# Token-stationary down products of an expert: high parts of four blocks first, their low parts behind

## Chip, cores, metric

One core of a Trainium2 chip runs one program. The metric is device microseconds of one execution; the kernel before takes 435.81 us, the median of 3 runs (434.45 to 435.82).

## What is computed

A linear attention with a per-channel decay feeds a dense two-layer network with a leaky activation, and that feeds a top-1 mixture of 8 experts. The change lies in the last part:

```python
expert_idx = np.argmax(x @ w_gate, axis=1)            # 1536 tokens, 8 experts
...                                                   # up to capacity = 384 tokens an expert
h = np.maximum(np.einsum('ecd,edf->ecf', disp, w1), 0.0)   # d = 384, f = 1024
y = np.einsum('ecf,efd->ecd', h, w2)
out[i] = gate_w[i] * y[expert_idx[i], pos[i]]
```

With these inputs the experts are chosen by 478, 132, 159, 141, 398, 57, 118 and 53 tokens. The first 256 rows of expert 0 are done ahead (the "early" rows), so the expert loop has 128 rows for expert 0, then 132, 159, 141, 384, 57, 118 and 53.

## The kernel before, in words

Every operand of a product is split into a high part (rounded) and a low part (the rest), and a product is three: high by high, high by low, low by high. `wh` and `wl` hold both parts of the weights (W1 in the first 384 columns of a slot, W2 in the other 384; 16 slots, so two experts' worth), `egh` and `egl` those of the hidden activations g.

An expert runs in tiles of 128 tokens, and the number of its rows decides, by branches on every engine, which code runs:

- **One tile** (experts 0, 5, 6, 7): "flipped". `flip_up` (L1604 to L1619) keeps the tokens stationary and gives h by token, 512 columns at once, in two halves; VectorE takes the relu (`flip_relu`, L1190); `flip_turn` (L1622 to L1635) transposes four blocks a half; ScalarE copies them as `egh` (`flip_high`, L843) and VectorE writes `egl` (`flip_low`, L1196, which for tile 0 raises `s_mgl` by four).
- **Two tiles** (experts 1, 2, 3): `expert_ups` (L1555) gives h by channel for 256 tokens in eight steps f, ScalarE takes the relu (`relu`, L790), VectorE the low part (`relu_low`, L1138). Then `expert_down` for tile 1 and for tile 0.
- **Three tiles** (expert 4): the same for tiles 0 and 1, and the third tile flipped.

`expert_down` (L1576 to L1597) is the down product of one tile: for each of the eight blocks f three matmuls of 384 columns, all of one accumulation in one PSUM bank. A block waits for its low part (`s_mgl`, or `s_fl` for the third tile) and for W2's low part (`s_wl2`).

TensorE's program for an expert has two branches one after the other: L1653 (one tile, or else) and L1674 (no third tile, or else). In the first arm of the second branch TensorE also raises a mark for the third tile that is not there:

```python
expert_down(e, 0, range(HF + 1))
pe.wait_ge(s_mgl, e * NFE + NFE + C_MGL)
pe.sem_inc(s_ft[1], 2)
expert_down(e, 0, range(HF + 1, NFE))
```

`s_ft[1]` is "third tile transposed". ScalarE and VectorE run the third tile's copies for every expert of two or three tiles (`flip_high(e, 2)`, L843, waits for that mark; `flip_low(e, 2, half)` behind it), whether there is such a tile or not. Behind `flip_high(e, 2)` ScalarE's queue has, in order: eight copies of W1 of expert e+2 (`split_high1`, L798) with the three scaled copies of y among them (L828), and then the relus of expert e+1 (L790). GpSimd forms W1's low parts from those eight copies (L633) and raises `s_gone` (L643) behind them; VectorE takes the token numbers and gates of the next expert (`keep_meta`, L1159 and L1160), which wait for `s_gone`, and only then the next expert's `relu_low`, W2's low parts (L1145) and the rows of the expert after (`xe_low`, L1151). TensorE's next `expert_down(e, 1)` waits, through `turned`, for two of these `xe_low`, since tile 1's bank holds transposed rows till then.

Of the kernel before, what the change touches and what calls it, by code (L numbers as in the profile page):

```python
# [3 lines left out]
P = 128  # L4


def attention_moe_kernel(nc, att_rk, att_v, decay, bonus, chunks, alpha, w_gate, out, disp,
# [26 lines left out]
    NF = FF // P  # L34
    NFE = FE // P
    SLOTS = 2 * NFE
    assert NF == SLOTS and CAP == GT * P and CT == 6 and PAIRS == KC + 1 and D == KC * PAD and CT == 2 * GT
    W1 = KC * P
    CW = W1 + DM
# [10 lines left out]
    ET = 2  # L50
# [32 lines left out]
    wh = base.take("w_high", [P, SLOTS, CW], f32r)  # L83
    wl_from = base.at
    wl = base.take("w_low", [P, SLOTS, CW], f32r)
# [77 lines left out]
    egh = moe.take("expert_g_high", [P, NFE, CAP], f32r)  # L163
    egl = moe.take("expert_g_low", [P, NFE, CAP], f32r)
# [4 lines left out]
    with ctx:  # L169
        bank = [ctx.enter_context(nc.psum_tensor(f"bank{i}", [P, 512], f32)) for i in range(8)]  # L170

        def sem(name):
            return ctx.enter_context(nc.semaphore(name))
# [48 lines left out]
        s_wl2 = sem("w2_low_ready")  # L222
# [10 lines left out]
        s_step = sem("step_done")  # L233
# [29 lines left out]
        s_ayo = sem("early_y_copied")  # L263
# [7 lines left out]
        s_mgl = sem("moe_g_low_ready")  # L271
# [4 lines left out]
        s_fc = [sem(f"flipped_g_high_ready{i}") for i in (0, 2)]  # L276
        s_fl = sem("third_tile_g_low_ready")
        s_yzero = sem("y_out_zeroed")
        s_yd = [None] + [sem(f"moe_y_done{i}") for i in range(1, GT)]
# [3 lines left out]
        C_MGL, C_YO, C_ROWS, C_GONE = 4, GT, 1, 1  # L283
# [64 lines left out]
        HF = NFE // 2  # L348
# [905 lines left out]
        def _(pe):  # L1254
            mm = pe.matmul
# [9 lines left out]
            for a in range(PAIRS):  # L1265
                last = pe.transpose(bank[6][:, a * P:(a + 1) * P], pw[:, 0, a, 1:P + 1], ident[:, :])
# [190 lines left out]
            for i in range(ET):  # L1457
                for kc in range(KC):
                    last = pe.transpose(bank[i][:, kc * P:(kc + 1) * P], xe[:, 1, i, kc * P:(kc + 1) * P], ident[:, :])
# [3 lines left out]
            for i in range(GT):  # L1463
                for m, (a, w) in enumerate(((gh, wh), (gh, wl), (gl, wh))):
                    last = mm(bank[4 + i][:, 0:DM], a[:, (NF - 1) % 4, i * P:(i + 1) * P], w[:, NF - 1, W1:CW],
                              start=False, stop=m == 2)
# [65 lines left out]
            def x_bank_free(e, i):  # L1532

                if i < 2:
                    y_bank_free(e, GT - 1 - i)
                else:
                    pe.wait_ge(s_tel, e * GT + GT)

            def y_bank_free(e, i):

                pe.wait_ge(s_yo, (e - 1) * GT + Y_ORDER.index(i) + 1 + C_YO)
# [29 lines left out]
            def turned(e, i):  # L1571

                if i and e < E - 1:
                    pe.wait_ge(s_tel, (e + 1) * GT + GT - i)

            def expert_down(e, i, fs=range(NFE)):  # L1576

                if fs[0] == 0:
                    turned(e, i)
                    if e:  # L1580
                        y_bank_free(e, i)
                    else:
                        pe.wait_ge(s_ayo, ET)
                for f in fs:
                    s = e * NFE + f
                    if i == 2:

                        pe.wait_ge(s_fl, 2 * e + f // HF + 1)
                    else:
                        pe.wait_ge(s_mgl, s + 1 + C_MGL)  # L1590
                    pe.wait_ge(s_wl2, s + NF + 1)
                    for m, (a, w) in enumerate(((egh, wh), (egh, wl), (egl, wh))):
                        last = mm(bank[4 + i][:, 0:DM], a[:, f, i * P:(i + 1) * P], w[:, s % SLOTS, W1:CW],  # L1593
                                  start=f == 0 and m == 0, stop=f == NFE - 1 and m == 2)
                    if i == 0:
                        last.then_inc(s_step, 1)
                if i and fs[-1] == NFE - 1:  # L1597
                    last.then_inc(s_yd[i], 1)

            def no_tile(i):  # L1600

                pe.sem_inc(s_yd[i], 1)

            def flip_up(e, i, half):  # L1604

                slot = e * NFE % SLOTS + half * HF
                w1_ready(pe, e, half * HF + HF - 1)
                if i:
                    pe.wait_ge(s_tel, e * GT + GT)

                    pe.wait_ge(s_mgl, e * NFE + HF + half + 1 + C_MGL)
                elif e:
                    pe.wait_ge(s_mgl, (e - 1) * NFE + HF + half + 1 + C_MGL)
                    flip_banks_free(e, half)
                for kc in range(KC):
                    for m, (x, w) in enumerate(((xeh, wh), (xeh, wl), (xel, wh))):
                        last = mm(bank[half][:, :].rearrange("p (f n) -> p f n", f=HF),  # L1617
                                  x[:, e % 2, kc, i * P:(i + 1) * P], w[:, slot:slot + HF, kc * P:(kc + 1) * P],
                                  start=kc == 0 and m == 0, stop=kc == KC - 1 and m == 2)  # L1619
                last.then_inc(s_fh[i // 2], 1)  # L1620
# [31 lines left out]
            for e in range(E):  # L1652
                with pe.If(rows[e] < P + 1):  # L1653
                    pe.wait_ge(s_tel, e * GT + GT - 1)
                    pe.sem_inc(s_mh, NFE)
                    for half in range(2):
                        flip_up(e, 0, half)
                        if e == 0 and half == 0:
                            turn_xe(0, 2, bank[6])
                    flip_turn(e, 0, (0,))  # L1660
                    if e < E - 1:
                        for i in range(GT):
                            if e:
                                x_bank_free(e, i)
                            turn_xe(e + 1, i, bank[X_BANK[i]])
                    flip_turn(e, 0, (1,))
                    no_tile(1)
                with pe.Else():
                    pe.wait_ge(s_tel, e * GT + GT - 1)
                    pe.sem_inc(s_fh[0], 2)  # L1670
                    pe.sem_inc(s_ft[0], 2)
                    expert_ups(e, 2 * P)
                    expert_down(e, 1)
                with pe.If(rows[e] < 2 * P + 1):  # L1674
                    pe.sem_inc(s_w1free, 1)
                    pe.sem_inc(s_fh[1], 2)
                    no_tile(2)
                    expert_down(e, 0, range(HF + 1))

                    pe.wait_ge(s_mgl, e * NFE + NFE + C_MGL)  # L1680
                    pe.sem_inc(s_ft[1], 2)
                    expert_down(e, 0, range(HF + 1, NFE))
                with pe.Else():
                    for half in range(2):
                        flip_up(e, 2, half)
                    pe.sem_inc(s_w1free, 1)
                    expert_down(e, 0, range(HF))
                    flip_turn(e, 2)
                    expert_down(e, 0, range(HF, NFE))
                    expert_down(e, 2)  # L1690


# [63 lines left out]
```

## Time and profile before

| | us |
|---|---|
| median of 3 runs | 435.81 |
| lowest, highest | 434.45, 435.82 |
| the profiled execution | 433.0 |
| its span, first to last instruction | 431.3 |
| TensorE busy in it | 407.6 (95%) |
| VectorE, ScalarE, GpSimd busy | 263.5, 195.5, 228.2 |
| matmuls of `expert_down`, L1593 | 312, by 335 to 342 ns |

The profiled execution is 2.8 us faster than the median; sums below are made against its own 433.0 us. Matmuls overlap each other, so that a matmul's own duration is about twice the distance from one start to the next.

### The profile page before, as it was taken

How to read it: one execution, taken by the hardware profiler on the slowest of the kernel's cores; microseconds unless marked ns; L12 is line 12 of the kernel's file. 1: busy time of each engine (PE TensorE's matmuls, PEld its weight loads, DVE VectorE, ACT ScalarE, POOL GpSimd, SP SyncE). 2: the span in 40 equal slices, each digit the busy share in tenths (PEclk: the TensorE clock that was granted, in tenths of full speed). 3: DMA queues.
4: the chain of work that ended last, by engine and by line, in shares of the span. 5: the costliest groups of instructions: out<-in, count | busy, mean ns of one | idle time of the engine just before them, and what ended most of it. 6: DMA issues, size and time to landing. Idle time of an engine off the chain costs nothing.

```text
span 431.3 us, 9203 instructions
## 1 busy us (share of the span) xinstructions
PE 407.6 (95%) x3200; PEld 389.3 (90%) x3200; DVE 263.5 (61%) x525; ACT 195.5 (45%) x446; POOL 228.2 (53%) x239
## 2 busy tenths in 40 slices
PE   5799999999999999999999999999699999999892
PEld 5698889999999999999999999987699999998672
DVE  6898867676436334353444796756586695726850
ACT  2889943433311114011142433425668777437840
POOL 3999725554322533126254593142939476437942
PEclk9999999999999999999999999999899999999997
DMA  6996035444990100001000455059575685817400
GB/s 244 403 370 217 3 82 165 131 135 152 362 358 3 53 2 0 0 0 55 0 0 4 129 154 171 18 144 388 176 254 161 234 258 185 277 25 244 140 29 10
DMA packets 34339, 61.89 MB, mean 144 GB/s; under 512 B 4798, under 2 KB 27310, under 8 KB 34288
## 3 DMA queue, kind: packets, MB, share of 16 engines
q1 hardware_dynamic: 31280, 55.92, 39.3%
q0 software_dynamic: 3008, 5.29, 3.6%
q8 instruction: 31, 0.51, 0.5%
q14 instruction: 20, 0.16, 0.1%
HBM read 47.92 MB, written 15.18 MB: 146 GB/s over the span
## 4 chain that ended last, share of the span: by engine, by line
PE 59%; PEld 15%; issue 7%; POOL 5%; DVE 5%; ACT 4%; DMA 2%; PEldq 0%; POOLq 0%; ACTq 0%; DVEq 0%
PE bank L1374 23%; PE bank L1359 23%; PEld bank L1593 7%; PEld bank L1555 6%; ACT scores L676 3%; POOL w_low L633 3%; PE bank L1480 2%; PE bank L1490 2%; DMA out<-y_out,token 2%; PEld bank L1617 1%; PE bank L1326 1%; DVE scores L956 1%; POOL out L609 1%; DVE w_low L1145 1%; PE bank L1617 1%
## 5 line engine op out<-in xcount | busy, mean ns | idle before, releaser
L551 POOL TENSOR_TENSOR g_low<-act_full,g_high 128x384 fp32r<-128x384 f32 x63 | 63.7, 1011 | 113.7 <-ACT g_high L705 113.7
L705 ACT ACTIVATE g_high<-act_full 128x384 fp32r<-128x384 f32 x64 | 33.7, 526 | 148.9 <-DVE act_full L1020 136.3
L1359 PE MATMUL bank<-x_split,w_high 128*128 (+1 forms) x384 | 98.3, 337 | 0.0
L1014 DVE TENSOR_SCALAR neg<-bank,alpha_sb 128x384 f32<-128x384 f32 x64 | 39.3, 614 | 78.0 <-PE bank L1359 78.0
L1359 PEld LDWEIGHTS bank<-x_split,w_high 128*128 128x128 f32 x384 | 69.0, 188 | 0.2 <-issue 0.2
L633 POOL TENSOR_TENSOR w_low<-w_raw,w_high 128x384 fp32r<-128x384 f32 x48 | 50.5, 1086 | 33.5 <-ACT w_high L798 33.5
L1374 PE MATMUL bank<-w_high,g_high 128*128 128x384 f32 x189 | 65.0, 344 | 0.0
L1359 PE MATMUL bank<-x_split,w_low 128*128 (+1 forms) x192 | 64.4, 336 | 0.0
L1374 PE MATMUL bank<-w_high,g_low 128*128 128x384 f32 x189 | 63.8, 338 | 0.0
L1374 PE MATMUL bank<-w_low,g_high 128*128 128x384 f32 x189 | 63.8, 337 | 0.0
L933 DVE TENSOR_TENSOR w_low<-w_raw,w_high 128x384 fp32r<-128x384 f32 x44 | 35.5, 812 | 10.5 <-ACT w_high L659 10.5
L1593 PE MATMUL bank<-w_high,expert_g_high 128*128 128x384 f32 x104 | 35.6, 342 | 2.9 <-DVE expert_g_low L1196 1.8
L1374 PEld LDWEIGHTS bank<-w_high,g_high 128*128 128x128 f32 x189 | 35.4, 187 | 2.1 <-POOL g_low L551 1.0
L1020 DVE SCALAR_TENSOR_TENSOR act_full<-bank,neg 128x384 f32<-128x384 f32 x64 | 35.7, 558 | 2.4
L1359 PEld LDWEIGHTS bank<-x_split,w_low 128*128 128x128 f32 x192 | 36.0, 188 | 0.0
L1374 PEld LDWEIGHTS bank<-w_low,g_high 128*128 128x128 f32 x189 | 35.5, 188 | 0.0
L1374 PEld LDWEIGHTS bank<-w_high,g_low 128*128 128x128 f32 x189 | 35.4, 187 | 0.0
L1593 PE MATMUL bank<-w_high,expert_g_low 128*128 128x384 f32 x104 | 34.8, 335 | 0.0
L1593 PE MATMUL bank<-w_low,expert_g_high 128*128 128x384 f32 x104 | 34.8, 335 | 0.0
L1145 DVE TENSOR_TENSOR w_low<-w_raw,w_high 128x384 fp32r<-128x384 f32 x48 | 33.0, 704 | 0.0
L609 POOL DMA_INDIRECT out<-y_out,token x24 | 26.0, 1082 | 12.5 <-DMA out<-y_out,token 6.7
L1555 PE MATMUL bank<-xe_high,w_high 128*128 128x256 f32 x96 | 28.5, 297 | 2.8 <-issue 2.8
(164 smaller groups left out, 846.3 us busy)
## 6 DMA issues: line engine op xcount, KB each, us to landing
w_raw<-chunks SPq DMA_DIRECT2D x96, 192.0 KB, 4.1
w_raw<-chunks SPq DMA_DIRECT2D x32, 384.0 KB, 3.5
rk_in<-att_rk SPq DMA_DIRECT2D x12, 704.0 KB, 6.4
routed_rows<-fill SPq DMA_DIRECT2D x1, 5211.0 KB, 16.8
xe<-routed_rows SPq DMA_DIRECT2D x7, 579.0 KB, 4.5
v_in<-att_v SPq DMA_DIRECT2D x12, 200.0 KB, 6.1
out<-fill SPq DMA_DIRECT2D x1, 2304.0 KB, 23.4
x_split<-x_split POOLq DMA_DIRECT2D x18, 48.0 KB, 2.5
```

The source lines that it names most:

```text
L551: pool.tensor_tensor(gl[:, f % 4, :], act_full[:, f % 2, :], gh[:, f % 4, :].bitcast(f32), ALU.subtract).then_inc(s_gl, 1)
L609: pool.indirect_dma_start(out=out, out_offset=bass.IndirectOffsetOnAxis(ap=token[:, e % 2, i:i + 1], axis=0), in_=y_out[:, e % 2, i, :], i ...
L633: pool.tensor_tensor(wl[:, slot, 0:W1], raw1[:, f, :], wh[:, slot, 0:W1].bitcast(f32), ALU.subtract).then_inc(s_wl1e, 1)
L705: act.activation(gh[:, f % 4, :], act_full[:, f % 2, :], ACT.Copy).then_inc(s_gh, 1)
L933: dve.tensor_tensor(wl[:, slot, part], raw[:, m, part], wh[:, slot, part].bitcast(f32), ALU.subtract).then_inc(s_wl1 if first else s_wl2, 1)
L1014: dve.tensor_scalar(neg[:, f % 2, :], h, 0.0, alpha_sb[:, f:f + 1], ALU.min, ALU.mult)\
L1020: dve.scalar_tensor_tensor(act_full[:, f % 2, :], h, 0.0, neg[:, f % 2, :], ALU.max, ALU.add)\
L1145: dve.tensor_tensor(wl[:, slot, W1:CW], raw2[:, f, :], wh[:, slot, W1:CW].bitcast(f32), ALU.subtract).then_inc(s_wl2, 1)
L1359: last = mm(bank[f % 4][:, 0:G], a[:, f, w], x[:, kc, bass.ds(g * G, G)], start=kc == 0 and i == 0, stop=kc == KC - 1 and i == 2)
L1374: last = mm(bank[4 + i][:, 0:DM], a[:, f % 4, i * P:(i + 1) * P], w[:, slot, W1:CW], start=f == 0 and m == 0, stop=f == n - 1 and m == 2)
L1555: last = mm(bank[f % 4][:, 0:n], a[:, slot, w], x[:, e % 2, kc, 0:n], start=kc == 0 and i == 0, stop=kc == KC - 1 and i == 2)
L1593: last = mm(bank[4 + i][:, 0:DM], a[:, f, i * P:(i + 1) * P], w[:, s % SLOTS, W1:CW], start=f == 0 and m == 0, stop=f == NFE - 1 and m == 2)
```

## The change

The down product of a flipped tile, and tile 0 of every expert without a third tile, is done by a new function in two halves of four blocks: first the eight matmuls with `egh` of the half, which wait for `s_fc` (the high part is copied), then the four with `egl`, which wait for `s_mgl` or `s_fl`. The mark `s_ft[1]` is raised behind the whole product and no longer behind its fifth block; the wait ahead of it is gone. `s_step`, which counts blocks done, is raised by the matmuls with `egl`.

```diff
+            def flip_down_high(e, i, half):
+                if half == 0:
+                    turned(e, i)
+                    if e:
+                        y_bank_free(e, i)
+                    else:
+                        pe.wait_ge(s_ayo, ET)
+                pe.wait_ge(s_fc[i // 2], 2 * e + half + 1)
+                for f in range(half * HF, (half + 1) * HF):
+                    s = e * NFE + f
+                    pe.wait_ge(s_wl2, s + NF + 1)
+                    for w in (wh, wl):
+                        mm(bank[4 + i][:, 0:DM], egh[:, f, i * P:(i + 1) * P], w[:, s % SLOTS, W1:CW],
+                           start=f == 0 and w is wh, stop=False)
+
+            def flip_down_low(e, i, half):
+                for f in range(half * HF, (half + 1) * HF):
+                    s = e * NFE + f
+                    if i == 2:
+                        pe.wait_ge(s_fl, 2 * e + half + 1)
+                    else:
+                        pe.wait_ge(s_mgl, s + 1 + C_MGL)
+                    last = mm(bank[4 + i][:, 0:DM], egl[:, f, i * P:(i + 1) * P], wh[:, s % SLOTS, W1:CW],
+                              start=False, stop=f == NFE - 1)
+                    if i == 0:
+                        last.then_inc(s_step, 1)
+                if i and half:
+                    last.then_inc(s_yd[i], 1)
+
+            def flip_down(e, i):
+                for half in range(2):
+                    flip_down_high(e, i, half)
+                    flip_down_low(e, i, half)
...
                     pe.sem_inc(s_w1free, 1)
                     pe.sem_inc(s_fh[1], 2)
                     no_tile(2)
-                    expert_down(e, 0, range(HF + 1))
-
-                    pe.wait_ge(s_mgl, e * NFE + NFE + C_MGL)
+                    flip_down(e, 0)
                     pe.sem_inc(s_ft[1], 2)
-                    expert_down(e, 0, range(HF + 1, NFE))
                 with pe.Else():
                     for half in range(2):
                         flip_up(e, 2, half)
...
                     expert_down(e, 0, range(HF))
                     flip_turn(e, 2)
                     expert_down(e, 0, range(HF, NFE))
-                    expert_down(e, 2)
+                    flip_down(e, 2)
```

How TensorE's rows stand at the first place, the arm without a third tile of an expert after the first: before, each block of three matmuls has its own two waits (`waits` names the semaphores).

```order
L1674 COMPARE_AND_BRANCH
L1593 MATMUL bank<-w_high,expert_g_high 128x384 [waits w2_low_ready,moe_g_low_ready,moe_y_copied]
L1593 MATMUL bank<-w_low,expert_g_high 128x384
L1593 MATMUL bank<-w_high,expert_g_low 128x384
L1593 MATMUL bank<-w_high,expert_g_high 128x384 [waits w2_low_ready,moe_g_low_ready]
```

Six more blocks follow like the last. The same place with the change:

```order
L1711 COMPARE_AND_BRANCH
L1613 MATMUL bank<-w_high,expert_g_high 128x384 [waits w2_low_ready,flipped_g_high_ready0,moe_y_copied]
L1613 MATMUL bank<-w_low,expert_g_high 128x384
L1613 MATMUL bank<-w_high,expert_g_high 128x384 [waits w2_low_ready]
L1613 MATMUL bank<-w_low,expert_g_high 128x384
L1613 MATMUL bank<-w_high,expert_g_high 128x384 [waits w2_low_ready]
L1613 MATMUL bank<-w_low,expert_g_high 128x384
L1613 MATMUL bank<-w_high,expert_g_high 128x384 [waits w2_low_ready]
L1613 MATMUL bank<-w_low,expert_g_high 128x384
L1625 MATMUL bank<-w_high,expert_g_low 128x384 [waits moe_g_low_ready] x4
```

The low parts are now asked for behind eight matmuls of a half; the second half is built alike. The raise of `s_ft[1]` is no row here (only waits and raises of a semaphore stand in such an instruction): it stood behind the fifth block's third matmul, with nine matmuls after it, and now stands behind the 24th.

The second place is the third tile of expert 4, whose first half now reads:

```order
L1613 MATMUL bank<-w_high,expert_g_high 128x384 [waits flipped_g_high_ready2,w2_low_ready,early_y_copied,xe_low_ready]
L1613 MATMUL bank<-w_low,expert_g_high 128x384
L1613 MATMUL bank<-w_high,expert_g_high 128x384 [waits w2_low_ready]
L1613 MATMUL bank<-w_low,expert_g_high 128x384
L1613 MATMUL bank<-w_high,expert_g_high 128x384 [waits w2_low_ready]
L1613 MATMUL bank<-w_low,expert_g_high 128x384
L1613 MATMUL bank<-w_high,expert_g_high 128x384 [waits w2_low_ready]
L1613 MATMUL bank<-w_low,expert_g_high 128x384
L1625 MATMUL bank<-w_high,expert_g_low 128x384 [waits third_tile_g_low_ready] x4
```

It waited for `third_tile_g_low_ready` ahead of its first matmul; the number of matmuls is the same. (The rows are those of expert 0's copy of this arm, which names `early_y_copied` where expert 4's names `moe_y_copied`.)

## Rows read from the trace of the kernel before

**Rows 1.** The page: the span, and the busy time of each engine.
```profile
span 431.3 us, 9203 instructions
...
PE 407.6 (95%) x3200; PEld 389.3 (90%) x3200; DVE 263.5 (61%) x525; ACT 195.5 (45%) x446; POOL 228.2 (53%) x239
```

**Rows 2.** Waits of TensorE, 289 to 431 us: total us, times, longest.
```profile
PE bank L1555 <- issue: 2.8, 1, 2.8
PE bank L1593 <- DVE expert_g_low L1196: 1.8, 4, 0.7
PE bank L1617 <- issue: 1.2, 1, 1.2
PE bank L1593 <- DVE w_low L933: 1.1, 1, 1.1
```

**Rows 3.** Waits of ScalarE, 289 to 431 us.
```profile
ACT expert_g_high L843 <- PEq L1681: 8.2, 3, 2.8
```

**Rows 4.** Waits of VectorE, 289 to 431 us.
```profile
DVE token L1159 <- POOLq L643: 20.2, 6, 6.4
```

**Rows 5.** Timeline of TensorE, experts 2 and 3: start, us, engine, line, operation.
```profile
335.95 0.42 PE L1593 MATMUL bank<-w_high,expert_g_high 128*128 128x384 f32 x1
...
344.36 0.28 PE L1555 MATMUL bank<-xe_high,w_high 128*128 128x256 f32 x1
...
348.92 0.36 PE L1555 MATMUL bank<-xe_high,w_high 128*128 128x256 f32 x1
...
353.63 0.49 PE L1522 MATMUL bank<-ident,xe 128*128 128x128 f32 x3
353.88 0.42 PE L1593 MATMUL bank<-w_high,expert_g_high 128*128 128x384 f32 x1
```

**Rows 6.** Timeline of ScalarE, the same stretch; in brackets the idle time before.
```profile
339.87 1.09 ACT L843 ACTIVATE expert_g_high<-bank 128x512 fp32r<-128x512 f32 x2 [2.73 <-PEq L1681]
340.84 1.77 ACT L798 ACTIVATE w_high<-w_raw 128x384 fp32r<-128x384 f32 x4
```

**Rows 7.** Timeline of GpSimd, the same stretch.
```profile
341.45 8.19 POOL L633 TENSOR_TENSOR w_low<-w_raw,w_high 128x384 fp32r<-128x384 f32 x8 [5.59 <-ACT w_high L798]
```

**Rows 8.** Timeline of VectorE, the same stretch.
```profile
345.36 1.06 DVE L1159 CAST token<-xe 128x3 int32<-128x3 f32 x1 [3.57 <-POOLq L643]
346.34 1.07 DVE L1160 COPY gate<-xe 128x3 f32<-128x3 f32 x1
347.31 0.41 DVE L1138 SCALAR_TENSOR_TENSOR expert_g_low<-bank,expert_g_high 128x256 fp32r<-128x256 f32 x1
...
353.18 0.55 DVE L1151 TENSOR_TENSOR xe_low<-bank,xe_high 128x384 fp32r<-128x384 f32 x1
```

**Rows 9.** Timeline of TensorE, first down matmul of experts 0 and 6.
```profile
298.35 0.41 PE L1593 MATMUL bank<-w_high,expert_g_high 128*128 128x384 f32 x1 [0.19 <-DVE expert_g_low L1196]
...
408.56 0.41 PE L1593 MATMUL bank<-w_high,expert_g_high 128*128 128x384 f32 x1 [0.68 <-DVE expert_g_low L1196]
```

**Rows 10.** Timeline of VectorE, expert 6: the low part of its first half.
```profile
407.78 0.68 DVE L1196 TENSOR_TENSOR expert_g_low<-bank,expert_g_high 128x512 fp32r<-128x512 f32 x1
```

**Rows 11.** The chain that ended last: start, us, what.
```profile
398.59 0.54 ACT w_high L798
...
399.20 3.80 POOL w_low L633 x4
...
417.67 4.32 DMA out<-y_out,token
```

**Rows 12.** Timeline of the last 7.3 us: the last scaled copy and the last scatter.
```profile
423.72 0.58 ACT L828 ACTIVATE y_out<-bank,gate 128x384 f32<-128x384 f32 x1 [3.54 <-PE bank L1593]
...
425.43 0.97 POOL L609 DMA_INDIRECT out<-y_out,token  x1 [0.31 <-issue]
```

**Rows 13.** Stretches: PE, PEld, DVE, ACT, POOL busy, then TensorE's granted clock, DMA share, GB/s.
```profile
307.00:318.00 11.00, 11.00 (x81) 11.00 (x82) 8.07 (x16) 6.48 (x17) 8.88 (x9) 0.84 0.79 245
401.00:412.00 11.00, 9.82 (x55) 8.68 (x56) 9.89 (x17) 9.00 (x21) 10.23 (x10) 1.00 0.25 77
```

## The prediction

> **What bounds the kernel now.** I read the page first: TensorE is busy for 407.6 of a span of 431.3 us [rows 1], so the program goes by TensorE wherever it isn't made to wait. The waits of TensorE in the expert loop are next [rows 2]. The reader should see how small they are: 1.8 us over four places for the low part of a flipped tile (L1196), which is what the new order goes around, and about 5 us of other waits that no operand explains. The four places are the one-tile experts, 0.19, 0.27, 0.68 and 0.66 us in the order 0, 5, 6, 7; two of them stand in [rows 9].
>
> Then the waits of the other engines, since the change also moves a mark that they wait for. ScalarE waits three times, 8.2 us in all, for TensorE's queue at L1681, the raise of `s_ft[1]` [rows 3]. The three are experts 1, 2 and 3. VectorE waits six times for GpSimd's `s_gone` [rows 4]. From the two views I followed one expert in the timelines.
>
> **The chain behind the mark.** Tile 1's down product of expert 2 starts at 335.95, its 48 matmuls (tiles 1 and 0) last until the next expert's first up product at 344.36 [rows 5]: 8.41 / 48 = 0.175 us each. ScalarE gets the mark and starts at 339.87 [rows 6], 3.92 us after the first of the 48, when the array is at the 22nd. The mark stands behind the 39th (24 of tile 1, 15 of tile 0): TensorE's queue handles semaphores some 17 matmuls ahead of the array. From there it goes from engine to engine without a gap:
>
> - ScalarE: two junk copies at 339.87, W1 copies from 340.84 [rows 6];
> - GpSimd: the low parts of W1 from 341.45 [rows 7];
> - VectorE: released by GpSimd at 345.36, two small copies of about 1 us each, the first `relu_low` at 347.31, and from there on busy without idle time to the second `xe_low`, 353.18 to 353.73 [rows 8];
> - TensorE: the next expert's tile 1 at 353.88, by 0.15 us later, right behind its last transpose at 353.63, so without a stall [rows 5].
>
> So 335.95 to 353.88, 17.93 us, is TensorE's own pace, and the chain through the other three engines takes 3.92 + 13.86 + 0.15, the same 17.93. It has almost no slack. The shortest way from a VectorE result to the matmul that waits for it is 408.46 to 408.56, 0.10 us [rows 9, 10], which leaves 0.05 us.
>
> **The change, part by part.**
>
> 1. *The mark, experts 1, 2 and 3.* It moves behind nine more matmuls: 9 x 0.175 = 1.58 us later, if TensorE's queue keeps its lead of some 17 matmuls; nothing in the new order blocks it there, for all low parts of such a tile are long written. Everything queued behind it is late by 1.58 us: the two junk copies, W1's copies, the copies of y and the relus on ScalarE; W1's low parts and `s_gone` on GpSimd; `keep_meta`, `relu_low`, W2's low parts and `xe_low` on VectorE. VectorE has no idle time in the chain to make it up, and its slow small copies beside GpSimd stay beside it, since both shift alike. Who waits first: the fifth up product, at 348.92 [rows 5], needs the first `relu_low`, now done at 347.31 + 0.41 + 1.58 = 349.30 [rows 8], some 0.4 us of stall with the semaphore; later stalls in the same chain are contained in the last. The last: tile 1's down product can start at 353.73 + 1.58 + 0.10 = 355.41, not 353.88: **+1.53 us**. The next expert's mark goes by this later start, so it adds up: three times (the starts of experts 2, 3 and 4), **+4.6 us**. Bounds of this term: nothing, if the lead of the queue grew by the nine matmuls, and 3 x 1.58 = 4.7. I take 4.6, since the rows of the chain show no room but 0.05 us.
> 2. *Flipped tiles, experts 0, 5, 6, 7.* The first eight matmuls start after ScalarE's copy and not after VectorE's difference: they save 1.8 us of waits in all [rows 2]. Of these only expert 0's 0.19 us [rows 9] is on the path. From expert 5 on the end is set elsewhere: ScalarE's W1 copies at 398.59, GpSimd's eight low parts from 399.20, then scatters and their landing, 417.67 and 4.32 us, before the last three scatters [rows 11]. TensorE's last tile is copied at 423.72 to 424.30 and its scatter starts only at 425.43, 1.1 us after [rows 12]. So 0.27 + 0.68 + 0.66 us cost nothing now and bring nothing. Expert 0's 0.19 stands ahead of two stalls of 1.1 and 2.8 us [rows 2], which may end at a time of their own; between 0 and -0.19 I take **-0.1**.
> 3. *Expert 4's third tile.* Its low parts are ready before TensorE comes to them (no wait on `s_fl` in the view), so nothing. The cover is tile 0's last twelve matmuls, 2.1 us.
> 4. *Order within a half.* The same 24 matmuls and 24 weight loads, the same bank: nothing. W2's low part of the fourth block is asked for three matmuls earlier, 0.5 us, and no wait of the view is for it in these tiles but the 1.1 us of expert 0 (put down to L933), whose operands are older. `s_step` of the first blocks comes up to 1 us later; its readers are the copies of later experts, which are not near it.
> 5. *Waits.* One per block and matmul group instead of two: TensorE's queue has some 12 instructions less for an expert. Where the array is fed 17 matmuls ahead that is hidden: nothing. If the queue ran dry it would be a gain.
>
> Sum: 4.6 - 0.1 = +4.5 us. The profiled execution would be 433.0 + 4.5 = 437.5; on the median, 435.8 + 4.5 = **440.3 us**.
>
> **The rivals.**
>
> *The mark is late by less* (0.14). The lead of the queue may be counted in instructions and not in matmuls: with fewer waits in the way it is longer by two or three matmuls, or there is some slack in the chain that I don't see. Then each of the three steps is about 0.9 us: 435.8 + 2.7 - 0.1 = 438.4. For it: the lead is inferred from one offset. Against: the offset is the same 3.92 to 3.93 us at all three experts.
>
> *Instruction fetch moves* (0.06). TensorE stands 2.8 us at the first up product of expert 1 and 1.2 us at that of expert 6 with no operand missing ("issue") [rows 2], both right behind a taken branch. The code up to expert 0's second branch is unchanged and behind it some 12 instructions an expert shorter, so one such stall can appear or go: 440.3 less or plus 1.2 to 2.8, 437.5 to 443.1. The Trainium skill, "Runtime: NRT & Kernel Launch", section "Instruction fetch mechanics", has this mechanism: instructions come in blocks of 256, and a taken branch out of the blocks at hand costs a fetch. By that rule a program that is shorter moves its branch targets against the blocks; the trace agrees that stalls sit at some branches and not at others.
>
> *Nothing happens* (0.08). The chain is late but ends in time, because the queue's lead had room: 435.8 - 0.1 = 435.7. Against it stands that the chain and TensorE's own pace agree to 0.05 us, and that ScalarE idles 2.7 us before the mark.
>
> *Faster* (0.05). If the mark's lateness is harmless and the end of the kernel goes by TensorE after all (the last scatters are late only because the landing of expert 6's took 4.32 us), the removed waits count in full: 435.8 - 1.8 = 434.0. It decides from the point where those scatters land more than 1.1 us sooner [rows 11, 12].
>
> *The clock falls* (0.07). After the 1.1 and 2.8 us of standing before expert 1 the granted clock is 0.84 over 307 to 318 us, that is, a part of it at 1.2 GHz for 2.4, some 1.8 us lost; in 401 to 412 us, with waits of 0.7 and 1.2 us, it stays at 1.00 [rows 13]. The new stalls are about 0.4, 0.3 and 0.8 us an expert, nearer to the second. If each dropped the clock: 440.3 + 3 x 1.8 = 445.7.
>
> **How the numbers follow.** My forecast has 0.60. A measurement of this kernel tells about 0.3% (1.3 us) from no change. Slower by more: 0.60 + 0.14 + 0.07 + 0.05 of the fetch case = 0.86. Within it: 0.08 and 0.01 = 0.09. Faster: 0.05. The range 437.0 to 443.0 holds the forecast with its bounds, the smaller step and the fetch case; it leaves out no change, faster, and the clock, together 0.20.
>
> **What would show it.** Right: ScalarE's first junk copy 5.5 us after the first down matmul of experts 1, 2, 3 (3.92 now); the distance between first down matmuls of experts 1 to 4 at 19.5 us (17.93 now); new waits of TensorE on `relu_low` (L1138) and `xe_low` (L1151), 1.5 us an expert; the waits on L1196 gone; VectorE busy without idle time between `keep_meta` and the flipped relus. Wrong: that distance still at 17.93, or a mark at 3.9 us. A span longer by 4.5 us with that distance unchanged would mean that the reason is another.

## The result, and the profile after

The changed kernel takes 438.69 us, the median of 4 runs (438.30 to 439.43), against 435.33 for the kernel before (4 runs, 434.45 to 435.82): the ratio is 1.0089, 95% interval 1.0068 to 1.0109, so 3.9 us slower by the ratio (3.0 to 4.7) and 3.4 by the medians. The forecast was slower by 4.5 us, 440.3, with a range of 437.0 to 443.0. The profiled execution took 438.3 us.

The page of the kernel after, against [rows 1]:

```profile
span 436.5 us, 9155 instructions
...
PE 411.1 (94%) x3200; PEld 391.2 (90%) x3200; DVE 262.9 (60%) x525; ACT 193.9 (44%) x446; POOL 228.3 (52%) x239
```

No engine has more work: the matmuls are 3200 as before. The 48 instructions less are put down to waits of TensorE's queue, which come to six for each expert. (The ends of matmuls are modelled, so the readings below go by starts.)

The waits of ScalarE, 289 to 437 us, against [rows 3]:

```profile
ACT expert_g_high L843 <- PEq L1716: 12.3, 3, 4.3
```

It waits for the mark, three times, 4.1 us longer in all than before. Then one expert, as in [rows 5 to 8]. TensorE, experts 2 and 3:

```profile
338.46 0.45 PE L1593 MATMUL bank<-w_high,expert_g_high 128*128 128x384 f32 x1 [0.43 <-issue]
...
346.90 0.28 PE L1555 MATMUL bank<-xe_high,w_high 128*128 128x256 f32 x1
...
352.00 0.36 PE L1555 MATMUL bank<-xe_high,w_high 128*128 128x256 f32 x1 [0.30 <-DVE expert_g_low L1138]
...
356.99 0.49 PE L1522 MATMUL bank<-ident,xe 128*128 128x128 f32 x3
357.89 0.44 PE L1593 MATMUL bank<-w_high,expert_g_high 128*128 128x384 f32 x1 [0.41 <-DVE xe_low L1151]
```

ScalarE in the same stretch:

```profile
343.96 1.09 ACT L843 ACTIVATE expert_g_high<-bank 128x512 fp32r<-128x512 f32 x2 [3.97 <-PEq L1716]
344.94 1.76 ACT L798 ACTIVATE w_high<-w_raw 128x384 fp32r<-128x384 f32 x4
```

GpSimd:

```profile
345.55 4.96 POOL L633 TENSOR_TENSOR w_low<-w_raw,w_high 128x384 fp32r<-128x384 f32 x5 [7.09 <-ACT w_high L798]
```

VectorE:

```profile
349.45 1.09 DVE L1159 CAST token<-xe 128x3 int32<-128x3 f32 x1 [3.57 <-POOLq L643]
350.46 1.07 DVE L1160 COPY gate<-xe 128x3 f32<-128x3 f32 x1
351.44 0.41 DVE L1138 SCALAR_TENSOR_TENSOR expert_g_low<-bank,expert_g_high 128x256 fp32r<-128x256 f32 x1
...
357.30 0.54 DVE L1151 TENSOR_TENSOR xe_low<-bank,xe_high 128x384 fp32r<-128x384 f32 x1
```

Read it as a distance from the first down matmul, 338.46: junk copy at 5.50 us (3.92 before), GpSimd at 7.09 (5.50), `keep_meta` at 10.99 (9.41), first `relu_low` at 12.98 (11.36), end of the second `xe_low` at 19.38 (17.78), next first down matmul at 19.43 (17.93). Each link in the other engines is 1.6 us later and no link is longer; TensorE's next down product is 1.5 us later. The stalls lie where the forecast put them. By the starts TensorE loses 0.55 us before the fifth up product (351.20 to 352.00, where 348.67 to 348.92 stood before), 0.2 before the sixth, and 0.65 before the down product. The idle times in brackets, 0.30 and 0.41, are shorter, because a matmul's modelled end lies behind the usual start of the next one. The forecast had 0.4, 0.3 and 0.8.

The whole difference of the two spans, 5.2 us, goes into pieces by the starts of TensorE's instructions:

| piece | before | after | difference |
|---|---|---|---|
| start to expert 0's second transposes | 297.56 | 297.83 | +0.27 |
| to expert 1's first up product | 9.38 | 9.34 | -0.04 |
| to its first down matmul | 11.08 | 11.87 | +0.79 |
| three experts, to expert 4's first down matmul | 53.79 | 58.29 | +4.50 |
| to the end of the span | 59.49 | 59.17 | -0.32 |

The third piece is the clock after the stalls of expert 0. The stretch 307 to 319 us of the kernel after:

```profile
307.00:319.00 12.00, 11.83 (x80) 11.86 (x81) 6.88 (x15) 6.21 (x17) 9.00 (x9) 0.78 0.81 258
```

The granted clock there is 0.78, for 0.86 in the same stretch before, a mix of 1.2 and 2.4 GHz in both. The same piece took 11.07 to 11.83 us in the experiments below, with 11.83 in one that has the old order, so the pair of profiles does not show it to be the change's. Without it the pair of profiles differs by 4.4 us.

### The profile page after: what moved, and what is told of

The parts are those of the page before. It is cut to its first block, busy times and chain, and to the rows that moved or that the text cites. A ratio compares the mean times of both kernels' runs of the same rounds, so it can differ in the third digit from the quotient of the medians.

```text
span 436.5 us, 9155 instructions
## 1 busy us (share of the span) xinstructions
PE 411.1 (94%) x3200; PEld 391.2 (90%) x3200; DVE 262.9 (60%) x525; ACT 193.9 (44%) x446; POOL 228.3 (52%) x239
## 4 chain that ended last, share of the span: by engine, by line
PE 66%; DVE 8%; POOL 6%; issue 6%; ACT 5%; PEld 4%; DMA 2%; ACTq 0%; POOLq 0%; PEldq 0%; DVEq 0%
PE bank L1374 23%; PE bank L1359 23%; POOL w_low L633 4%; ACT scores L676 3%; PEld bank L1593 2%; PE bank L1480 2%; PE bank L1555 2%; DVE w_low L1145 2%; PE bank L1593 2%; PE bank L1654 2%; PE bank L1490 2%; DMA out<-y_out,token 1%; PE bank L1326 1%; DVE scores L956 1%; PE bank L1613 1%
## 5 line engine op out<-in xcount | busy, mean ns | idle before, releaser
L633 POOL TENSOR_TENSOR w_low<-w_raw,w_high 128x384 fp32r<-128x384 f32 x48 | 50.5, 1092 | 38.9 <-ACT w_high L798 38.9
L676 ACT ACTIVATE scores<-ident,diag 128x128 f32<-128x128 f32 x96 | 29.3, 394 | 2.3 <-DVE diag L948 2.3
L1555 PE MATMUL bank<-xe_low,w_high 128*128 128x256 f32 x96 | 28.2, 293 | 0.0
L1555 PE MATMUL bank<-xe_high,w_low 128*128 128x256 f32 x96 | 28.1, 293 | 0.0
```

Source lines behind the costliest of these rows:

```text
L633: pool.tensor_tensor(wl[:, slot, 0:W1], raw1[:, f, :], wh[:, slot, 0:W1].bitcast(f32), ALU.subtract).then_inc(s_wl1e, 1)
L676: last = act.activation(scores[:, t % 2, h % 2, h // 2, :], ident[:, :], ACT.Copy, scale=diag[:, t % 2, h:h + 1])
L1555: last = mm(bank[f % 4][:, 0:n], a[:, slot, w], x[:, e % 2, kc, 0:n], start=kc == 0 and i == 0, stop=kc == KC - 1 and i == 2)
```

## The experiments

Each experiment changes one or a few lines of the kernel before or of the kernel after. Theory A is the forecast: the late mark costs all of it, through ScalarE, GpSimd and VectorE. Theory B is that the order itself costs, and theory C that instruction fetch or the clock does. "Distance" is the time between the first down matmuls of neighbouring experts among 1 to 4.

### The new order with the mark where it was

```diff
                         mm(bank[4 + i][:, 0:DM], egh[:, f, i * P:(i + 1) * P], w[:, s % SLOTS, W1:CW],
                            start=f == 0 and w is wh, stop=False)
+                        if mark and f == HF + 1 and w is wh:
+                            pe.sem_inc(s_ft[1], 2)
...
-                    flip_down(e, 0)
-                    pe.sem_inc(s_ft[1], 2)
+                    flip_down_high(e, 0, 0)
+                    flip_down_low(e, 0, 0)
+                    flip_down_high(e, 0, 1, mark=True)
+                    flip_down_low(e, 0, 1)
```

> New order of the down products, but s_ft[1] raised behind the 15th matmul of tile 0, as before. Theory A (the late mark costs all of it): ScalarE's first junk copy 3.9 us after the first down matmul of experts 1, 2, 3; the distance between the first down matmuls of experts 1 to 4 is back at 17.93 us; 4.5 us less than with the whole change, 434 to 435.5 us, within 0.3% of before. Theory B (the order itself costs, by s_step that comes later or by waits for W2's low part): the distance stays at 19.4 us and the time at 438 to 439 us. Theory C (instruction fetch or clock by the shorter code): the distance is 17.93 but the time is over 437 us.

Measured: 435.35 us (12 runs), ratio 1.0002 (0.9982 to 1.0021). TensorE, then ScalarE:

```profile
318.40 0.42 PE L1593 MATMUL bank<-w_high,expert_g_high 128*128 128x384 f32 x1
...
336.33 0.42 PE L1593 MATMUL bank<-w_high,expert_g_high 128*128 128x384 f32 x1
```

```profile
322.34 1.09 ACT L843 ACTIVATE expert_g_high<-bank 128x512 fp32r<-128x512 f32 x2 [2.75 <-PEq L1616]
```

Mark at 3.94 us, distances 17.93 and 17.97, then 18.96. In that third distance VectorE's small copy of the token numbers, which is 1.07 us long at the other experts, took 4.04 us. The first `relu_low` began 2.1 us later for it, and TensorE stood 0.78 us before an up product:

```profile
363.72 4.04 DVE L1159 CAST token<-xe 128x3 int32<-128x3 f32 x1 [3.57 <-POOLq L643]
```

So the last distance is the same chain made longer by something else than the mark. The new order alone costs nothing and brings nothing that these runs tell (0.8 us slower or 0.9 faster at most, by the interval): B and C fall as causes of the 3.9 us.

### The old order with the late mark

```diff
-                    expert_down(e, 0, range(HF + 1))
-                    pe.wait_ge(s_mgl, e * NFE + NFE + C_MGL)
-                    pe.sem_inc(s_ft[1], 2)
-                    expert_down(e, 0, range(HF + 1, NFE))
+                    expert_down(e, 0)
+                    pe.sem_inc(s_ft[1], 2)
```

> The kernel before with one edit: s_ft[1] raised behind the 24th matmul of tile 0, in the old order; the wait ahead of the mark is gone too. Theory A: first junk copy 5.5 us after the first down matmul, distance 19.43 us, slower than before by 4.3 to 4.7 us, 439 to 440.5 us. Theory B: no change, 435 us, distance 17.93. Theory C: no change in the distance.

Measured: 439.47 us (6 runs), ratio 1.0094 (1.0069 to 1.0118), the same as the whole change. TensorE, then ScalarE:

```profile
320.02 0.42 PE L1593 MATMUL bank<-w_high,expert_g_high 128*128 128x384 f32 x1
...
339.41 0.44 PE L1593 MATMUL bank<-w_high,expert_g_high 128*128 128x384 f32 x1 [0.41 <-DVE xe_low L1151]
...
358.82 0.44 PE L1593 MATMUL bank<-w_high,expert_g_high 128*128 128x384 f32 x1 [0.42 <-DVE xe_low L1151]
```

```profile
325.52 1.09 ACT L843 ACTIVATE expert_g_high<-bank 128x512 fp32r<-128x512 f32 x2 [4.31 <-PE bank L1593]
```

Mark at 5.50 us, distances 19.39, 19.41 and 19.39. The two kernels together settle it: the mark is the cause, the order isn't. The mark comes at 5.50 us here, with two waits for each block in TensorE's queue, and at 5.50 us in the kernel after, with fewer.

### A smaller dose: the mark behind the 18th matmul, old order

```diff
-                    expert_down(e, 0, range(HF + 1))
+                    expert_down(e, 0, range(HF + 2))
...
-                    expert_down(e, 0, range(HF + 1, NFE))
+                    expert_down(e, 0, range(HF + 2, NFE))
```

> The kernel before with s_ft[1] raised behind the 18th matmul of tile 0 and not the 15th. Theory A: 3 x 0.175 = 0.52 us later, of which the chain's slack of some 0.05 to 0.1 us is taken first: distance 18.36 to 18.42 us, 1.3 to 1.5 us over before in all. A chain with more room than I saw: distance under 18.2.

Measured: one run, 436.81 us, so its trace counts and not its time. TensorE, then ScalarE:

```profile
319.82 0.42 PE L1593 MATMUL bank<-w_high,expert_g_high 128*128 128x384 f32 x1
...
338.21 0.44 PE L1593 MATMUL bank<-w_high,expert_g_high 128*128 128x384 f32 x1 [0.23 <-issue]
```

```profile
324.27 1.09 ACT L843 ACTIVATE expert_g_high<-bank 128x512 fp32r<-128x512 f32 x2 [3.27 <-PEq L1681]
```

Mark at 4.45 us, distances 18.39, 18.41, 18.40: three matmuls later cost 0.46 to 0.48 us an expert, of 0.52 by which the mark moved. The slack of the kernel before is the 0.05 us that the forecast read from it. From there to nine matmuls it is 1.0 us for 1.05.

### The new order with the mark ahead of the down product

```diff
+                    pe.sem_inc(s_ft[1], 2)
                     flip_down(e, 0)
-                    pe.sem_inc(s_ft[1], 2)
```

> New order, s_ft[1] raised ahead of tile 0's down product. Theory A: TensorE's own pace bounds the loop, so that an earlier mark than before brings nothing more: distance 17.93 us, first junk copy 1.3 us after the first down matmul or later, when ScalarE has done its relus and W2 copies; time as with the mark behind the 15th, within 0.5 us. If instead TensorE was paced by the chain even before, the distance falls below 17.9 and the time by up to 1 us. Theory B: as the whole change, 438 to 439 us.

Measured: 434.78 us (12 runs), ratio 0.9991 (0.9970 to 1.0012). TensorE, then ScalarE:

```profile
317.55 0.44 PE L1593 MATMUL bank<-w_high,expert_g_high 128*128 128x384 f32 x1
...
335.48 0.42 PE L1593 MATMUL bank<-w_high,expert_g_high 128*128 128x384 f32 x1
```

```profile
319.93 1.09 ACT L843 ACTIVATE expert_g_high<-bank 128x512 fp32r<-128x512 f32 x2 [0.86 <-PEq L1715]
```

The distance is 17.93 three times, so that is TensorE's own pace, and an earlier mark takes nothing off it. It does give the chain room: VectorE's token copy took 4.03 us at 325.42 in this execution too, and here it cost nothing, where it cost 1.0 us above. Another execution with the same order and mark (the second kernel of the tail, below) has 18.02, 18.10 and 18.09 us, since there `xe_low` ended only 0.05 us ahead of the down product. The mark comes at 2.38 us (1.9 to 2.1 at the next two experts), not at 1.3, and ScalarE did wait for it (0.86 us). So the lead of TensorE's queue is smaller at this place. It stands right behind a branch, but whether that is the reason was not tried.

### The link from ScalarE to VectorE: `s_gone` early, with the whole change

```diff
             for e in range(E):
+                if 0 < e < 4:
+                    pool.wait_ge(s_out, e * 16 * GT)
+                    pool.sem_inc(s_gone, 1)
                 if e + FIRST < E:
                     for f in range(NFE):
                         split_low1(e + FIRST, f)
-                if e:
+                if e > 3:
                     pool.wait_ge(s_out, e * 16 * GT)
                     pool.sem_inc(s_gone, 1)
```

> The whole change, and GpSimd raises s_gone ahead of the eight low parts of W1 and not behind them, for experts 1, 2 and 3. Theory A says which link carries the lateness from ScalarE to VectorE: keep_meta, which waits for s_gone. Without it the first relu_low starts right behind ScalarE's first relu, at 330.7 and not 332.0 us in the trace of the change, so 1.3 us of the 1.5 come back; but one more of VectorE's W2 differences runs beside GpSimd and takes 1.04 for 0.54 us. Distance between first down matmuls 18.2 to 18.7 us (19.43 now), time 2.2 to 3.6 us under the whole change, 435.3 to 437 us. If another link carries it (GpSimd's low parts, ScalarE's relus), the distance stays at 19.4.

Measured: 437.03 us (6 runs), ratio 1.0053 (1.0035 to 1.0071). VectorE, with lines 3 higher than before (L1141 is `relu_low`, L1148 W2's low part, L1154 `xe_low`):

```profile
331.29 0.42 DVE L1141 SCALAR_TENSOR_TENSOR expert_g_low<-bank,expert_g_high 128x256 fp32r<-128x256 f32 x1 [3.41 <-ACT expert_g_high L793]
331.70 1.41 DVE L1148 TENSOR_TENSOR w_low<-w_raw,w_high 128x384 fp32r<-128x384 f32 x1
...
338.05 0.54 DVE L1154 TENSOR_TENSOR xe_low<-bank,xe_high 128x384 fp32r<-128x384 f32 x1
```

The first down matmul of expert 1 is at 319.69 here, so `relu_low` starts 11.60 us after it, 12.96 in the kernel after: the 1.3 us came as expected. But the distance is 18.95 to 18.98, above the 18.2 to 18.7 expected, and only 0.47 us came back. Three of VectorE's W2 differences now run beside GpSimd's, 1.41, 1.05 and 1.04 us, where two did in the kernel after, 1.12 and 1.04, and the third took 0.54. So one more was hit, as expected, but with the longer first one it cost 0.8 us and not 0.5. `keep_meta` is the first link, and right behind it stands the second, VectorE beside GpSimd. The Trainium skill, "SBUF — State Buffer", section "SBUF: two separate sides", has a port pair of VectorE and GpSimd that one instruction holds while the other waits. The durations agree with it: 0.54 us alone, 1.04 beside an operation of about 1 us of GpSimd.

### The tail: no wait ahead of the last scatters

Three kernels drop GpSimd's wait for the landing of earlier scatters at the last expert. In the first nothing else is changed; the second has the new order and the mark ahead of it, the third the old order and the mark ahead of it.

```diff
-                if e:
+                if 0 < e < E - 1:
                     pool.wait_ge(s_out, e * 16 * GT)
                     pool.sem_inc(s_gone, 1)
```

> The kernel before, and GpSimd no longer waits, ahead of the last expert's three scatters, for the landing of the earlier ones (nobody reads s_gone after it). Theory A, tail by the scatters: in the profile before, the last scatter starts at 425.43, 1.1 us after its y is copied; without the wait the two scatters of the tiles that are not there go out before y is ready, and the last goes out right behind the copy: 0.9 to 1.1 us less, 434.2 to 434.4 us against 435.25. If the end went by TensorE anyway in most executions: no change within 0.3 us.

> The new order of the down products, s_ft[1] raised ahead of tile 0's down product, and no wait ahead of the last scatters. Theory A: the tail now goes by TensorE, so that the 0.6 to 0.7 us that expert 7's first down matmul no longer waits, and some of expert 6's, come to the end: 1.5 to 2 us under before, 433.3 to 433.8 us, and under the same without the new order by 0.6 to 1 us. If the new order brings nothing even here: equal to that one, within 0.2 us.

> The old order of the down products, s_ft[1] raised ahead of tile 0's down product, no wait ahead of the last scatters. Theory A: distance between the first down matmuls 17.93 us; time as the kernel with the last wait gone alone, 434.2 to 434.4 us; 0.6 to 1 us over the same with the new order.

Measured, 12 runs each: 434.67 us, ratio 0.9976 (0.9961 to 0.9992); 434.87, 0.9982 (0.9964 to 0.9999); 435.19, 0.9989 (0.9966 to 1.0012). The first gained 1.0 us by its ratio, the 0.9 to 1.1 that was expected; the second gained 0.8 where 1.5 to 2 were expected, and the third 0.5. The order makes no difference that the intervals tell. But the traces have no room for 1 us at this place. The first kernel's last copy of y (ScalarE) and last scatter (GpSimd):

```profile
425.09 0.58 ACT L828 ACTIVATE y_out<-bank,gate 128x384 f32<-128x384 f32 x1 [3.55 <-PE bank L1593]
```

```profile
426.47 0.97 POOL L609 DMA_INDIRECT out<-y_out,token  x1 [2.35 <-ACT y_out L828]
```

A scatter starts 0.8 us after the copy that it waits for has ended (425.67 to 426.47). So of the 1.1 us in [rows 12] only 0.3 were room. From expert 7's first down matmul to the end of the span it is 11.72 to 11.83 us in all traces without the wait, 12.12 in the kernel before, and 11.75 to 11.92 in the kernel after and the other kernels that keep the wait. So most executions have hardly any room there, and the 1.0 us isn't explained by the tail.

A fourth kernel joined the first with the early `s_gone`, in the old order:

> The kernel before, with s_gone raised early for experts 1 to 3 and no wait ahead of the last expert's scatters. Theory A: TensorE paces these experts already, so the distance stays at 17.93 us and the early s_gone gives nothing; what is gained is that of the last wait alone, 0.9976 of before as measured for it, 434.0 to 434.7 us where before is 435.1.

Measured: 434.55 us (12 runs), ratio 0.9998 (0.9985 to 1.0010), distances 17.92 to 17.94. The early `s_gone` indeed gives nothing, but the 0.2% of the missing last wait isn't there either. Its interval and that of the first kernel hardly meet, and the kernel before itself was at 435.59 us beside the one and at 434.65 beside the other. The intervals of the first two kernels lie under 1, but this fourth one, which has the first one's edit in it, is equal to before. The tail's 0.3 us is below what these runs can tell: no version here is shown to beat the kernel before.

### Does a flipped tile start sooner? The branches taken out

In the kernel after, the first down matmul of experts 6 and 7 stands as far behind the second transposes as before (1.31 and 1.32 us for 1.34 and 1.32), with the same idle time. TensorE, expert 7:

```profile
423.41 0.66 PE L1671 MATMUL bank<-ident,expert_g_by_token 128*128 128x128 f32 x4 [0.35 <-issue]
424.73 0.41 PE L1613 MATMUL bank<-w_high,expert_g_high 128*128 128x384 f32 x1 [0.66 <-issue]
```

ScalarE had copied that half long before, at 423.19 to 423.79:

```profile
423.19 0.60 ACT L843 ACTIVATE expert_g_high<-bank 128x512 fp32r<-128x512 f32 x1 [3.70 <-issue]
```

Between the two TensorE rows stand the jump over the first branch's other arm and the second branch's compare. Theory D is that these branches hold TensorE there, and theory L that the low part does, as the view of waits says. So two kernels put the down product of a one-tile expert into the first arm, behind the transposes, and the second branch into the other arm; the first on the tail's second kernel (new order), the second on its third (old order).

```diff
                     flip_turn(e, 0, (1,))
                     no_tile(1)
+                    pe.sem_inc(s_w1free, 1)
+                    pe.sem_inc(s_fh[1], 2)
+                    no_tile(2)
+                    pe.sem_inc(s_ft[1], 2)
+                    flip_down(e, 0)
                 with pe.Else():
...
                     expert_down(e, 1)
-                with pe.If(rows[e] < 2 * P + 1):
+                    with pe.If(rows[e] < 2 * P + 1):
```

In the old order the added product is `expert_down(e, 0)`.

> The kernel t2_order_mark0_no_last_wait with one more edit: in TensorE's program the down product of a one-tile expert stands in the first arm, right behind the second transposes, without the two branches between them. Measured by the distance from the second transposes to the first down matmul, which was 1.32 us at experts 6 and 7 in both orders. Theory D (the branches hold TensorE's queue there, not an operand): it falls to 0.45 to 0.7 us, since the high part is long copied; 0.6 to 0.8 us less at expert 7 and so at the end, 434 us. Theory L (the low part, or something with it, holds it as the view of waits says): it stays at 1.3 us, for the branch is not the reason. For expert 0 to 1 the taken branch is another one, so the stalls there can change by 1 us either way.

> The same edit on t3_mark0_no_last_wait, with the old order of the down products. Theory D: the branches are gone but the low part is now what ends last: VectorE ends it 1.15 to 1.2 us after the start of the second transposes and the matmul starts 0.1 us later, 1.25 to 1.32 us, so nothing is gained at experts 6 and 7; n1 is faster than this by 0.6 to 0.8 us at expert 7. Theory L: 1.3 us in both.

Measured: 439.27 us, ratio 1.0117 (1.0083 to 1.0152), and 441.14, ratio 1.0150 (1.0117 to 1.0183), 6 runs each. New order without the branches, TensorE:

```profile
308.77 0.55 PE L1555 MATMUL bank<-xe_high,w_high 128*128 128x256 f32 x1 [6.25 <-issue]
...
424.13 0.66 PE L1671 MATMUL bank<-ident,expert_g_by_token 128*128 128x128 f32 x4 [0.35 <-DVE expert_g_by_token L1190]
425.08 0.41 PE L1613 MATMUL bank<-w_high,expert_g_high 128*128 128x384 f32 x1 [0.29 <-issue]
```

Old order without the branches, TensorE, and VectorE's first half:

```profile
427.02 0.66 PE L1634 MATMUL bank<-ident,expert_g_by_token 128*128 128x128 f32 x4 [0.35 <-DVE expert_g_by_token L1190]
428.28 0.41 PE L1593 MATMUL bank<-w_high,expert_g_high 128*128 128x384 f32 x1 [0.61 <-DVE expert_g_low L1196]
```

```profile
427.49 0.69 DVE L1196 TENSOR_TENSOR expert_g_low<-bank,expert_g_high 128x512 fp32r<-128x512 f32 x1 [0.53 <-ACT expert_g_high L843]
```

From the second transposes to the first down matmul, in us:

| | expert 0 | 5 | 6 | 7 |
|---|---|---|---|---|
| before: old order, branches | 0.79 | 0.87 | 1.34 | 1.32 |
| after: new order, branches | 0.82 | 0.73 | 1.31 | 1.32 |
| old order, no branches | 0.79 | 0.79 | 0.79 | 1.26 |
| new order, no branches | 0.40 | 0.39 | 0.60 | 0.95 |

Each theory has half of it. At experts 0, 5 and 7 the low part and the branches end at nearly the same time: take the one away (the new order) or the other (the branches), and the distance stays within 0.14 us. Only with both gone does it fall, by 0.4 to 0.5 us, to 0.40, 0.39 and 0.95; at expert 7 0.45 to 0.7 was expected. Expert 6 is different. In the old order the branches' removal alone took it from 1.34 to 0.79 us, where 1.25 to 1.32 was expected. But VectorE began the low part together with the second transposes there (both at 415.24) and 0.56 us behind them in the kernel before (407.22 and 407.78), so that step isn't the branches' alone.

The whole is slower by the ratios: 5.1 and 6.5 us over the kernel before. TensorE stands 6.25 and 6.39 us before expert 1, for 2.8 before, while the stall of 1.1 us ahead of it is gone, so it is 2.3 to 2.5 us more in all. It stands 2.72 and 2.98 us before expert 6, for 1.2. The view puts these two down to GpSimd's low part of W1 (L633), but the parts that expert 6 needs were written by 396.0 and 396.6 us, more than 9 us earlier, and its rows (`xe_low`) by 401.8. Two stalls more are in both, 0.7 us between experts 2 and 3 and 1.3 to 1.45 before expert 7, all "issue". The clock takes a share too: over 405 to 412 us it is 0.76 and 0.56, for 1.00 in the two kernels that they were made from. The jump over the longer arm fits the first two stalls, but it was not tried apart from the nested branch. The Trainium skill, "Runtime: NRT & Kernel Launch", section "Instruction fetch mechanics", says that a taken branch out of the instructions at hand waits for a fetch. The trace agrees with a stall at these places and no operand missing; that it grows with the jump is what the two kernels show, not what the page says.

## Why the prediction was right, and where it wasn't

1. **The mark, +4.6 us.** Right, and shown from both sides by the old order with the late mark (1.0094) and the new order with the mark in its place (1.0002). It measured 4.50 us in the pair of profiles: distances 19.42, 19.43 and 19.44 for a forecast of 19.46, the mark at 5.50 to 5.52 us. What made it possible to size was one comparison: the chain through the other engines against TensorE's own pace, and the shortest gap from a result to its reader as the measure of slack. The dose of three matmuls gave that slack again as 0.05 us.
2. **Flipped tiles, "they save 1.8 us of waits in all".** Wrong, though the sum hardly felt it: the four waits were put down to L1196 and weren't its alone. Three of them are there in the kernel after, as "issue" or against an operand long written; at expert 7 the first down matmul comes 1.32 us behind the second transposes in both. What ends at the same time are the two branches between transposes and down product. At expert 5 the recorded wait is gone and the distance 0.14 us shorter; at the other three nothing came of it. The forecast counted 0.1 us of this on the path, and the piece at expert 0 gave 0.04, within what that piece varies by (8.85 to 10.70 us). That the sum came out near is luck in this term: the end of the kernel was taken to hide the other three, and there was nothing to hide.
3. **The tail, "1.1 us after".** The room was 0.3 us: 0.8 us pass between the end of a copy and the start of its scatter. In the kernel after, the last scatter already goes by the copy (ScalarE's, then GpSimd's last row), 0.80 us from the end of the one to the start of the other:

```profile
429.27 0.58 ACT L828 ACTIVATE y_out<-bank,gate 128x384 f32<-128x384 f32 x1 [3.54 <-PE bank L1625]
```

```profile
430.65 0.97 POOL L609 DMA_INDIRECT out<-y_out,token  x1 [0.61 <-issue]
```

4. **Third tile, order within a half, fewer waits: nothing.** Right; the new order with the mark in its place is equal to before. The waits that went are six for each expert and not some 12.
5. **The rivals.** No change and faster fell with the ratio. Instruction fetch did not move clear of what the pieces ahead of expert 1 vary by. (Its upper end, 443.1 us, lies 0.1 outside the range that was said to hold it.) The clock did not fall in the three experts: the new stalls are 0.3 to 0.4 us each in the record, 0.65 at most by the starts, and the granted clock over 319 to 400 us stays 1.00. The smaller lateness (438.4 us) is nearest to the measured median, but not its mechanism: the mark is late by the full 1.58 us. The forecast of 4.5 us lies within the interval of the ratio, 3.0 to 4.7 us; by the medians 1.1 us of it is missing, and no run settles why.

The traces have one candidate. Seven of the experiments' traces with branches have the mark no more than three matmuls late. In four of them (the marks behind the 15th and the 18th matmul, and the second and third kernel of the tail) VectorE's copy of the gates ahead of expert 6's relu took 1.07 us and not 0.15, and TensorE stood 1.0 us ahead of expert 6's second transposes; in the three with the mark nine matmuls late it never stood there for more than 0.23 us. The profiled execution of the kernel before, 433.0 us, is one without this stall. If many of its others have it, the late mark costs less by the medians than by the pair of profiles. Seven executions against three are too few to show that.

## What to carry to other kernels

A semaphore raised in an engine's queue between its instructions is work with a due time of its own: when a block of matmuls is reordered, look up who waits for every mark that moves with it, what is queued behind that waiter, and compare the length of the chain with the pace of the engine that bounds. Here the product that was to start sooner had its waits named by the profile after the operand that came last, while two branches ended at nearly the same time. Before a wait is designed away, ask what else ends within 0.1 us of it.

## What the runs showed of the hardware

- TensorE's queue handles a semaphore some 16.6 matmuls ahead of the array: the mark came at 3.92 to 3.94, 4.45 and 5.50 us, that is at the 22.4th, 25.4th and 31.4th matmul, when it stood behind the 39th, the 42nd and the 48th. With a weight load for each matmul that is 33 instructions. The Trainium skill, "TensorE: Matmul & The Clock Gate", section "Architectural detail: the array is 16× 32×32, not 1× 128×128", gives a queue of 64; these runs show half of that as the lead of a semaphore, and right behind a branch still less.
- A longer arm to jump over, with a nested branch in it, made the same jump cost 6.3 to 6.4 us for 2.8, and 2.7 to 3.0 for 1.2.
- VectorE's copies of 128x3 elements in the two-tile experts took 1.0 to 1.1 us beside GpSimd's operations of 1 us, where 0.15 is the shortest, and three times 3.05 to 4.04.
- Stalls of TensorE for about 1.5 us in 19.4 us, in pieces of 0.65 at most, left the granted clock at 1.00; 1.1 and 2.8 us with six matmuls between them brought it to 0.84 over the next 11 us [rows 13].
